# Local attention with a global key block: where the global keys and values are copied, and what the scores and weighings wait for

## What is computed

```python
s_g = scale * np.matmul(q_g, k_all.transpose(0, 1, 3, 2))      # global queries see all 544 keys
out_g = np.matmul(sm(s_g), v_all)
s_ll = scale * np.matmul(q_l, k_l.transpose(0, 1, 3, 2))       # local queries: keys within 32 ...
mask = np.abs(pos[:, None] - pos[None, :]) <= 32
s_ll = np.where(mask, s_ll, -1000000000.0)
s_lg = scale * np.matmul(q_l, k_g.transpose(0, 1, 3, 2))       # ... and the 32 global keys
a_l = sm(np.concatenate([s_lg, s_ll], axis=-1))
out_l = np.matmul(a_l, np.concatenate([v_g, v_l], axis=2))
```

## Time and profile before

| | us |
|---|---|
| median of 3 runs | 663.09 |
| lowest, highest | 660.63, 668.54 |
| the profiled execution | 662.77 |
| its span in the trace | 661.0 |
| TensorE busy | 589.3 |
| VectorE, ScalarE, GpSimd busy | 320.4, 277.3, 87.1 |

### The profile page before, as it was taken

The page is one execution under the profiler, slowest core; times in us unless marked ns, Lnnn a source line. Parts: engine busy times, 40 slices in busy tenths (PEclk is TensorE's granted clock), DMA queues, the critical chain, the costliest instruction groups (busy, mean ns, idle before and its releaser), DMA issues. The chain is left out here.

```text
span 661.0 us, 17698 instructions
## 1 busy us (share of the span) xinstructions
PE 589.3 (89%) x7124; PEld 493.2 (75%) x7124; DVE 320.4 (48%) x773; ACT 277.3 (42%) x735; POOL 87.1 (13%) x173
## 2 busy tenths in 40 slices
PE   5778656878888899989979998989999999999998
PEld 4566545666686578769759767879989898898986
DVE  4356533647715534553571674765434353443512
ACT  3457433648935533643553453634132241312311
POOL 1000000002416511320332321200000000000000
PEclk9989867979999789989999988999999999999999
DMA  9986993895112100000000000300000000000000
GB/s 171 189 181 116 202 192 60 166 185 102 31 33 92 53 1 2 1 1 0 0 0 17 1 1 1 129 33 1 32 0 32 16 16 32 0 32 16 17 33 16
DMA packets 97535, 36.38 MB, mean 55 GB/s; under 512 B 89152, under 2 KB 92480, under 8 KB 97472
## 3 DMA queue, kind: packets, MB, share of 16 engines
q1 hardware_dynamic: 97472, 35.47, 25.8%
HBM read 27.54 MB, written 4.46 MB: 48 GB/s over the span
## 5 line engine op out<-in xcount | busy, mean ns | idle before, releaser
L44 PE MATMUL ps_H<-XH,w_kL 128*128 128x256 f32 (+1 forms) x288 | 81.5, 283 | 1.2 <-ACT square L1499 1.2
L45 PE MATMUL ps_H<-XL,w_kH 128*128 128x256 f32 (+1 forms) x288 | 81.1, 282 | 0.0
L46 PE MATMUL ps_H<-XH,w_kH 128*128 128x256 f32 (+1 forms) x288 | 81.0, 281 | 0.0
L1499 ACT ACTIVATE square<-ps_H 128x512 f32<-128x512 f32 (+1 forms) x36 | 20.5, 573 | 142.4 <-PE ps_H L46 139.9
L44 PEld LDWEIGHTS ps_H<-XH,w_kL 128*128 128x128 f32 x288 | 54.9, 191 | 2.2 <-ACT square L1499 1.4
L44 PE MATMUL ps_V<-w_vH,HL 128*128 128x512 f32 x136 | 53.1, 391 | 2.3 <-DVE HL L1551 2.3
L45 PEld LDWEIGHTS ps_H<-XL,w_kH 128*128 128x128 f32 x288 | 54.9, 191 | 0.4
L46 PEld LDWEIGHTS ps_H<-XH,w_kH 128*128 128x128 f32 x288 | 54.9, 190 | 0.0
L45 PE MATMUL ps_V<-w_vL,HH 128*128 128x512 f32 x136 | 53.0, 390 | 0.0
L46 PE MATMUL ps_V<-w_vH,HH 128*128 128x512 f32 x136 | 53.0, 390 | 0.0
L604 DVE TENSOR_TENSOR probs<-ps_S,mask 128x512 f32<-128x512 f32 x32 | 22.1, 691 | 54.4 <-PE ps_S L400 54.4
(11 more groups left out here) (242 smaller groups left out, 1464.9 us busy)
## 6 DMA issues: line engine op xcount, KB each, us to landing
VW<-in_v_l_dram SPq DMA_DIRECT2D x32, 336.0 KB, 6.3
out_dram<-gate SPq DMA_DIRECT2D x17, 256.0 KB, 2.0
QKn<-in_k_l_dram SPq DMA_DIRECT2D x32, 128.0 KB, 3.4
QKn<-in_q_l_dram SPq DMA_DIRECT2D x32, 128.0 KB, 3.3
VW<-VW SPq DMA_DIRECT2D x8, 422.5 KB, 6.9
raw_b<-in_moe_w_k_dram SPq DMA_DIRECT2D x8, 256.0 KB, 2.8
raw_c<-in_moe_w_v_dram SPq DMA_DIRECT2D x6, 256.0 KB, 2.8
raw_b<-in_moe_w_r_dram SPq DMA_DIRECT2D x4, 256.0 KB, 2.6
```

Source lines behind the costliest of these rows:

```text
L44: nc.tensor.matmul(out, al, bh, start=(starts and k == 0), stop=False)
L45: nc.tensor.matmul(out, ah, bl, start=False, stop=False)
L46: last = nc.tensor.matmul(out, ah, bh, start=False, stop=(ends and k == n - 1))
```

## The change

The global block goes to the end of each row of 128 keys: the global values of a window lie in partitions 96 to 127, and masks, maxima and the order of the global queries' chunks follow. GpSimd instead of a DMA spreads the global values over the windows (`spread_vg`: one TENSOR_TENSOR for window 1, one copy for windows 2 to 13). A new tile KB, in one allocation with KS, holds each key block beside the global one; GpSimd fills it for each pair (`string_keys`, two instructions). Scores then take one matmul of 128 columns: two key blocks from KS and two (the third block and the global one) from KB. KB has two places, used by turns. Scores wait for GpSimd's string (`k_strung`), the first weighing of a half for GpSimd's spread (`vg_spread`), and the first weighing of each pair for that pair's two value loads. Weight splits are taken in GpSimd's steps, between the new work. SyncE issues by pair, and in batch 0 the values of pair 0 come ahead of the keys and queries of pair 1.

```diff
...
+        ones = m.sbuf("ones", [P, 1])
+        KK = m.sbuf("KK", [P, 4 * SL + 4 * SL])
+        KS = KK[:, 0:4 * SL].rearrange("p (a s) -> p a s", a=4)
+        KB = KK[:, 4 * SL:8 * SL].rearrange("p (a n k s) -> p a n k s", a=2, k=2, s=SG)
         GT = m.sbuf("GT", [P, 2, 2, SG])
         GQ = m.sbuf("GQ", [P, 2, 2, 2, SG])
...
-        most, rest = probs_g[:, 1:6, SG:P], probs_g[:, 0:2, :].rearrange("p c k -> p (c k)")[:, P - SG:P + SG]
+        most, rest = probs_g[:, 0:5, 0:P - SG], probs_g[:, 5, P - 2 * SG:P]
...
-        v_loaded, vg_loaded, vg_copied = ([M.sem(f"{kind}{i}") for i in range(2)] for kind in ("v_loaded", "vg_loaded", "vg_copied"))
+        vg_loaded = [M.sem(f"vg_loaded{i}") for i in range(2)]
+        vg_spread, k_strung = M.sem("vg_spread"), M.sem("k_strung")
+        v_loaded = [M.sem(f"v_loaded{i}") for i in range(4)]
...
-        G_LOADS, K_LOADS, Q_LOADS, V_LOADS, RAW_LOADS = 2, 2, 2, 4, 5
-        IDENTITIES, MASKS, POOL_SET = 4, 8, 9
+        G_LOADS, K_LOADS, Q_LOADS, V_LOADS, RAW_LOADS = 2, 2, 2, 2, 5
+        IDENTITIES, POOL_SET = 4, 10
...
+        SPREAD_AT = {5: (0, 1), 11: (1, 0)}
...
-                def load_qk(b, hf):
+                def load_qk(b, pair):
                     if b:
-                        sp.wait_ge(q_turned, 4 * b - 4 + 2 * hf + 2)
-                    for pair in range(2):
-                        for kind, loc, loaded in ((1, kl_h, k_loaded), (0, ql_h, q_loaded)):
...
-                def load_v(b, hf):
+                        sp.wait_ge(q_turned, 4 * b - 4 + 2 * (pair // 2) + 2)
+                    for kind, loc, loaded in ((1, kl_h, k_loaded), (0, ql_h, q_loaded)):
+                        for n in (2 * (pair % 2), 2 * (pair % 2) + 1):
+                            h = H * b + 4 * (pair // 2) + n
+                            sp.dma_start(QKn[:, pair // 2, kind, :, n, :],
+                                         loc[h:h + 1, :, :].rearrange("h (j p) d -> p (h j) d", p=P)
...
+                def load_v(b, pair):
+                    hf = pair // 2
                     if b:
                         sp.wait_ge(weighed, UB * b - UB + UH * hf + UH)
                     h = H * b + 4 * hf
-                    sp.dma_start(VW[0:SG, hf, 0, :, 0:DH], vg_h[h:h + 4, :, :].rearrange("h p d -> p h d")).then_inc(vg_loaded[hf], 16)
-                    for n in range(4):
+                    if pair % 2 == 0:
+                        sp.dma_start(VW[P - SG:P, hf, 0, :, 0:DH], vg_h[h:h + 4, :, :].rearrange("h p d -> p h d")
+                                     ).then_inc(vg_loaded[hf], 16)
...
 
...
-                        sp.dma_start(VW[SG:P, hf, :, n, 0:DH],
-                                     bass.AP(v.tensor, v.offset, [[DH, P - SG], [SG * DH, NW], [1, DH]])).then_inc(v_loaded[hf], 16)
-
-                def copy_vg(b, hf):
-
-                    sp.wait_ge(pool_set, POOL_SET)
-                    sp.wait_ge(vg_loaded[hf], 16 * (b + 1))
-                    sp.dma_start(VW[0:SG, hf, 1:NW, :, :].rearrange("p w h d -> p w (h d)"),
-                                 VW[0:SG, hf, 0, :, :].rearrange("p h d -> p (h d)").unsqueeze(1)
-                                 .to_broadcast([SG, NW - 1, 4 * VD])).then_inc(vg_copied[hf], 16)
+                        sp.dma_start(VW[0:P - SG, hf, :, n, 0:DH],
+                                     bass.AP(v.tensor, v.offset, [[DH, P - SG], [SG * DH, NW], [1, DH]])
+                                     ).then_inc(v_loaded[pair], 16)
 
                 load_g(0)
                 load_qk(0, 0)
+                sp.wait_ge(pool_set, POOL_SET)
                 load_v(0, 0)
                 load_qk(0, 1)
-                copy_vg(0, 0)
                 load_v(0, 1)
-                copy_vg(0, 1)
+                for pair in (2, 3):
+                    load_qk(0, pair)
+                for pair in (2, 3):
+                    load_v(0, pair)
                 for b in range(1, B):
                     load_qk(b, 0)
+                    load_qk(b, 1)
                     load_g(b)
-                    load_qk(b, 1)
-                    load_v(b, 0)
-                    copy_vg(b, 0)
-                    load_v(b, 1)
-                    copy_vg(b, 1)
...
                                         pattern=[[-SG, 4], [-1, SG]], channel_multiplier=1).then_inc(pool_set, 1)
+                nc.gpsimd.memset(ones[:], 1.0).then_inc(pool_set, 1)
                 nc.gpsimd.memset(VW[:, :, :, :, DH:VD], 1.0).then_inc(pool_set, 1)
...
-                for n in range(len(pieces)):
-                    split_weights(n)
+                def string_keys(b, pair):
+                    hf = pair // 2
+                    pool.wait_ge(k_kept, 4 * b + pair + 1)
+                    pool.wait_ge(g_kept, 2 * b + hf + 1)
+
+                    spread = 2 * b + (0, 1, 1, 2)[pair]
+                    if due(b, pair):
+                        pool.wait_ge(vg_spread, spread)
+
+                    before = 5 * (hf - 1) + 2 * (pair % 2) + 2
+                    if due(b, before):
+                        pool.wait_ge(scored, 10 * b + before)
+                    nc.gpsimd.tensor_tensor(KB[:, pair % 2, 2:, 1, :], GT[:, hf, pair % 2, :].unsqueeze(1).to_broadcast([P, NW, SG]),
+                                            ones[:].unsqueeze(2).to_broadcast([P, NW, SG]), ALU.mult)
+                    nc.gpsimd.tensor_copy(KB[:, pair % 2, 2:, 0, :], KS[:, pair, 2 * SG:SL].rearrange("p (n s) -> p n s", s=SG)
+                                          ).then_inc(k_strung, 1)
+
+                def spread_vg(b, hf):
+                    pool.wait_ge(vg_loaded[hf], 16 * (b + 1))
+                    pool.wait_ge(k_strung, 4 * b + (1, 3)[hf])
+                    if isinstance(b, int) and b == B - 1 and hf == 1:
+                        pool.wait_ge(w_split, split_at(b, 5)[-1] + 1)
+                    if due(b, 0):
+                        pool.wait_ge(weighed, UB * b - UB + UH * hf + UH)
+                    first = VW[P - SG:P, hf, 0, :, :].rearrange("p h d -> p (h d)")
+                    rows = VW[P - SG:P, hf, :, :, :].rearrange("p w h d -> p w (h d)")
+                    nc.gpsimd.tensor_tensor(rows[:, 1, :], first, ones[P - SG:P, :].to_broadcast([SG, 4 * VD]), ALU.mult)
+                    nc.gpsimd.tensor_copy(rows[:, 2:NW, :], first.unsqueeze(1).to_broadcast([SG, NW - 2, 4 * VD])
+                                          ).then_inc(vg_spread, 1)
+
+                def step(b, i):
+                    turn_at(b, i, K_AT, string_keys)
+                    for n in split_at(b, i):
+                        split_weights(n)
+                    turn_at(b, i, SPREAD_AT, spread_vg)
+
+                turn_at(0, -1, K_AT, string_keys)
+                spread_vg(0, 0)
+                run(pool, step, 0)
...
-                        pe.wait_ge(k_kept, 4 * b + pair + 1)
-                        pe.wait_ge(g_kept, 2 * b + hf + 1)
+                        pe.wait_ge(k_strung, 4 * b + pair + 1)
...
                     for n in range(2):
-                        for local in (True, False):
-                            for k in range(4):
-                                s = 4 * (2 * t + n) + k
-                                at = SG * window(s)
-                                for r in range(2):
-                                    rows = slice(64 * r, 64 * r + 64)
-                                    q = QT[rows, pair % 2, SG * s:SG * s + SG]
-                                    out = ps_S[SG * k:SG * k + SG, r, P * n:P * n + P]
-                                    if local:
-                                        nc.tensor.matmul(out[:, SG:P], q, KS[rows, pair, at:at + P - SG], start=True, stop=True)
-                                    else:
-                                        last = nc.tensor.matmul(out[:, 0:SG], q, GT[rows, hf, pair % 2, :], start=True, stop=True)
+                        for k in range(4):
+                            s = 4 * (2 * t + n) + k
+                            w = window(s)
+                            own = SL * pair + SG * w
+                            beside = 4 * SL + 2 * SL * (pair % 2) + 2 * SG * (w + 2)
+                            for r in range(2):
+                                rows = slice(64 * r, 64 * r + 64)
+                                q = QT[rows, pair % 2, SG * s:SG * s + SG]
+                                two = KK[rows, own:own + 2 * SG]
+                                keys = bass.AP(two.tensor, two.offset, [list(two.ap[0]), [beside - own, 2], [1, 2 * SG]])
+                                last = nc.tensor.matmul(ps_S[SG * k:SG * k + SG, r, P * n:P * n + P], q, keys,
+                                                        start=True, stop=True)
...
                     pe.wait_ge(pt_kept, UB * b + u + 1)
+                    if v < 4 and t == 0:
+                        pe.wait_ge(v_loaded[pair], 16 * V_LOADS * (b + 1))
                     if v == 0:
```

(7 more changed lines are left out.)

24 lines of the change are left out of this document (12 added, 12 removed).

## The result

On the chip on which both were first timed, the changed kernel took 640.69 us (median of 4 runs, 635.49 to 650.26) against 664.79 for the kernel before: a ratio of 0.961, 95% interval [0.951, 0.972]. On another chip, in a later set of runs, the same two took 647.85 and 658.95: 0.978 [0.973, 0.984]. The change is faster in both, by 24 us in the first and by 11 in the second.

What follows compares the result with a forecast made beforehand. SyncE's load chain and the DMA engines, with TensorE, were taken to bound the first three batches. Copies 9.7, scores 1.9, fetch wait 0.7, less 1.0 for the last batch, make 11.3 off 662.8: 651.5 us, range 641 to 659.

Steps and rivals of the forecast that it cites:

- The copy up to 42.1 us: Before the globals wait ending at 42.09 us, dropping two DMA copies of global values saves 3.6 us (2.5 to 4.9).
- 61.3 to 89.4: In this stretch, with DMA engines full, dropping the copy of global values saves 2.0 us.
- The branch: At the loop's return from batch 1 to 2, TensorE's 6.41 us wait shrinks by 2.1 us (0 to 6.4).
- Small fetch waits: Inside a block of scores, a 0.71 us TensorE wait taken for late instructions goes: 0.7 us (0 to 2.8).
- Up to 135.5: In the stretch ending at 135.5 us, where TensorE waited 2.62, dropping the copy saves 2.0 us.
- Scores in one matmul: Score blocks with 32 records instead of 64 save 0.15 us each, over about 13 blocks: 1.9 us.
- Strings and spreads: GpSimd's key strings take 1.9 us per pair and value spreads 4.0 per half, hidden except in the last batch.
- Last batch: Spread and string after the eighth weight split make scores 2.0 us late; counted as a 1.0 us loss (0 to 6).
- Does a busy GpSimd slow VectorE?: On VectorE beside GpSimd's new work: no slowing, from mask additions of 692 ns with GpSimd idle and 690 at work.
- the gain is larger: Rival: branch and small fetch waits mostly go and TensorE keeps its clock; 643.4 us, chance 0.14.
- the transfer was hidden anyway: Rival: the copy's rows pass beside others, so only SyncE's issue time counts; 658.5 us, chance 0.16.
- GpSimd as the path: Rival: GpSimd decides when a spread takes over some 12 us; kernel slower at 679 us, chance 0.08.

Runs made afterwards that it cites:

- run a1: One more execution of the changed kernel, nothing altered, against the kernel before; it took 648.3 us.
- one-operand form: Changed kernel with VectorE's last global minimum as a reduction over one two-column operand: 640.46 us, 0.971 of the kernel before; attention ends at 162.5.
- the best version: Changed kernel with raw weights loaded later, the earlier start order, last spread ahead of weight splits and one-operand minimum: 631.92 us, 0.960 of the kernel before.

## Why the prediction was right and wrong

Taken by the steps of the sum, on the profiled executions of the kernels before and after (24.3 us less span, forecast 11.3):

- *The copy up to 42.1 us:* forecast 3.6, the wait to end at 38.5. It came to 37.40 without a wait: 4.7. Right, near the upper end by bytes (4.9).
- *61.3 to 89.4:* forecast 2.0; the stretch is 1.4 shorter. Right in size; here the raw weights, not the copy, are what is long: of SyncE's issues those five take 11.1 us.
- *The branch:* forecast 2.1 of 6.4, because "what shares the engines with it ends 2.1 us sooner". **This is the step that failed.** The wait went whole, and with it more of the stretch: 8.2. The condition was wrong, not only the size. The prediction counted the records that merged scores save and priced their own time and one small fetch wait; that fewer of them could spare the loop its fetch altogether wasn't asked. Two-part scores bring 6.19 us back with no copy by DMA in the kernel, and merged scores leave it out with that copy there.
- *Small fetch waits:* forecast 0.7 for one, ends 0 and 2.8. The prediction read six waits in the earlier trace rows and missed that of 2.39 us at 77.73 and smaller ones. Eight of them, 6.31 us, went with the records; they come back with two-part scores (4.8 us). Some of it is hidden, since TensorE then waits longer for globals.
- *Up to 135.5:* forecast 2.0; 3.7. The copy, four shorter score blocks (0.9) and three fetch waits that went (0.41, 0.43 and 0.75) all fall here; their shares aren't parted.
- *Scores in one matmul:* forecast 0.15 us a block, ends 0 and 0.22. At full clock a block now takes 0.60 us from start to start and took 0.83:

```profile
47.40 0.67 PE L442 MATMUL ps_S<-KK,QT 64*32 64x128 f32 x32
48.00 0.66 PE L457 MATMUL ps_P<-ident,probs_g 128*128 128x128 f32 x4
```

  0.23 is just past the upper end, 0.22, but not for its reason. The working took 0.60 us for the old block from the rates of its first 32 records; the whole block of the earlier trace rows goes from 165.27 to 166.10, 0.83. And records don't cost the same: one of 128 columns takes 0.60/32 = 19 ns, one of 96 took 12. At the low clock I had 0; there a block took 1.23 us (92.17 to 93.40 in the kernel before) and takes 1.04 (95.44 to 96.48 in run a1), so 0.19 is saved there too. The stretch from 42.09 has 1.8 us less and that from 135.51 2.6; I had 2.6 for scores and small fetch waits in the whole kernel.
- *Strings and spreads:* 1.5 and 3.4 us for 1.9 and 4.0, hidden but for the last batch and for what they do to VectorE (below). The two slopes give 4.2 and 2.9 us for the copy of 3120, not 4.1 and 2.8; it took 2.78.
- *Start:* a delay of 2 us before the 42 us chain, without cost. A wait of 4.26 us is there; no run shows that it costs anything later.
- *Last batch:* forecast 2.0 us late for the string, -1.0 in all. The string ended at 149.72 (GpSimd's rows: 149.17 + 0.55) and TensorE went on at 149.82, after 2.28 us; the profile names VectorE, whose work had ended at 149.03. The stage is 2.1 us longer, where 1.0 was forecast. Right in place, half in size: with it VectorE's split of XL took 2.73 us for 0.71, since it met the spread, which I had not priced.
- *"Does a busy GpSimd slow VectorE?"* I read mask additions, which read PSUM, and left the rule for two SBUF inputs at "no row here bears it out or denies it", without looking which instructions of the kernel have two such inputs. There are two kinds, the minimum and the split of XL, and the first stands between the maxima and the exponentials. This is a loss that the sum had at nothing: 7.4 us between the medians of the kernel after and of its one-operand form in the same set, 4.7 by the ratios.
- *The rest of the kernel:* forecast unchanged. It is 4.1 us shorter in this pair of traces, but over the others it takes 469.4 (copy in four pieces) to 475.6 (the best version), and 471.5 in the kernel before, unrolled, whose code there is the same as in the kernel before. So these 4.1 us are no gain that is shown. The rest goes for the most part with its granted clock: 0.97 where it takes 473.7 us and more, 0.98 or 0.99 where it takes less. Three of the four traces at 0.97 are those with the raw weights loaded late, so an effect of that edit isn't ruled out.

So two errors of opposite sign: too little at the branch, nothing for VectorE. In the profiled execution the second hardly fell due (one long minimum, the first). In the trace of the second set it fell due twice more, and the medians of that set are 11.1 us apart, about what I had forecast: that is luck, two errors that cancel. Of the rivals, "the gain is larger" (643.4) had the branch wait go; it held that wait and the small ones to stand for busy DMA engines, but with the copy by DMA put back the branch wait stays away. That the transfer was hidden anyway falls with the DMA copy put back: attention then ends at 174.2, against 162.5 for the kernel without VectorE's stands, though that run has none of them either. That is 11.7 us for the copy between two traces, 9.2 by the ratios of the two runs (0.985 and 0.971), forecast 9.7. By the same counts two-part scores cost 17.8 us (180.2; no long minimum there either) and 12.2 by the ratios. In the traces the two add up to 29.5, more than the 22.9 between the kernel before and that one. Either edit shifts the same waits for globals, which may be why they don't add up; no run parts this.

GpSimd as the path did not come: spreads take 3.4 us, not 12.

What stays open: how many instructions TensorE holds; and what sets off the drops of the granted clock in the rest of the kernel, which go with up to 6.2 us from one trace to another.

## What to carry to other kernels

Count a loop body's instructions per engine before and after a change: here a body that no longer had to be fetched again lost its wait at the branch whole, and unrolling instead only spread that wait. When work moves to GpSimd, list VectorE's instructions with two SBUF operands and its bf16 copies within SBUF, and see whether GpSimd can run beside them. The minimum was cured by giving it one operand, or by cutting GpSimd's instruction short. A meeting cost the rest of GpSimd's instruction here, and about twice that where TensorE's granted clock fell behind it. A kernel whose runs scatter by 2% with nothing else changed is worth two traces side by side.

## What the runs showed of the hardware

- A 128x1 minimum of VectorE with two SBUF operands took 0.16 us free and up to 2.75 while GpSimd copied 32x3120 floats (2.78 us): it ends with the copy. In four pieces it took at most 0.61. With one operand it took 0.15 to 0.16 always, inside the copy too. A bf16 copy of a mask (32x128), which has one operand, stood too, at the first spread; it took 0.19 us where a DMA made the spread, and others of its group took 0.18:

```profile
9.34 2.70 DVE L715 COPY mask<-above 32x128 bf16<-32x128 bf16 x1
```

- A stand of 2.7 us in what feeds TensorE was followed by 6 us at a granted clock of 0.50, and cost 5.8 us; stands of 2.4 and 2.5 us at the same place cost about 4.6.
- With 1477 records of TensorE a turn of the loop the instruction queue moved 2 packets a turn and TensorE didn't stand for them; with 1979 it moved 10, and TensorE stood 6.4 us at the branch.
